# Order of matrix products and helper work in the expert part of an attention and expert kernel on one Trainium2 core

## The reference

```python
def _moe_ref(x, w_gate, w1, w2):            # x (2304, 512), 8 experts, F = 1024
    logits = x @ w_gate
    logits = logits - logits.max()
    P = np.exp(logits)
    for _ in range(8):
        P /= P.sum(1, keepdims=True) + 1e-09
        P /= P.sum(0, keepdims=True) + 1e-09
        P *= N / E
    for e in range(E):
        h = np.maximum(x @ w1[e], 0.0)
        ye = h @ w2[e]
        out += P[:, e:e + 1] * ye
```

## Time and profile before

| | us |
|---|---|
| median of 3 runs (lowest, highest) | 1875.57 (1874.74, 1875.81) |
| the profiled execution: its time | 1877.03 |
| the profiled execution: its span | 1874.8 |
| TensorE busy (share of the span) | 1854.2 (99%) |
| weight loads, beside the matmuls | 1601.0 (85%) |
| GpSimd busy | 1077.7 (57%) |
| VectorE busy | 978.2 (52%) |
| ScalarE busy | 760.3 (41%) |
| granted TensorE clock, mean share of full speed | 0.997 |

### The profile page before, as it was taken

How to read it: one execution, slowest core, us unless ns; L and a number is a source line. 1 busy time by engine, 2 the same in 40 slices (tenths; PEclk the granted TensorE clock), 3 DMA queues, 4 the chain that set the end, 5 groups by cost and what they waited for, 6 DMA issues and landing times.

```text
span 1874.8 us, 27897 instructions
## 1 busy us (share of the span) xinstructions
PE 1854.2 (99%) x10255; PEld 1601.0 (85%) x10255; DVE 978.2 (52%) x1846; ACT 760.3 (41%) x1314; POOL 1077.7 (57%) x720
## 2 busy tenths in 40 slices
PE   8999999899999999999999999999999999999999
PEld 4677777688999999998999999999989999999998
DVE  8877777757543444346434443444464434444443
ACT  8776777433333333334333333333333333333332
POOL 0223225456766666666676666666666666666662
PEclk9999999999999999999999999999999999999999
DMA  7753451111111111112111111111122111111110
GB/s 246 219 148 90 126 150 46 45 48 65 68 68 68 67 68 68 68 68 102 67 68 68 68 68 68 68 67 68 68 102 68 68 68 68 68 68 68 68 68 34
DMA packets 44160, 152.55 MB, mean 81 GB/s; under 512 B 9594, under 2 KB 18042, under 8 KB 29710
## 3 DMA queue, kind: packets, MB, share of 16 engines
q1 hardware_dynamic: 44046, 151.04, 24.9%
HBM read 135.69 MB, written 15.34 MB: 81 GB/s over the span
## 4 chain that ended last, share of the span: by engine, by line
PE 94%; DVE 2%; issue 0%; ACT 0%; DVEq 0%
PE banks L646 14%; PE banks L645 14%; PE banks L644 14%; PE banks L612 12%; PE banks L614 12%; PE banks L616 12%; PE banks L525 5%; PE banks L486 4%; PE banks L468 3%; PE banks L469 2%; PE banks L551 1%; PE banks L496 0%; DVE h_lo L1116 0%; DVE x_lo_first L1021 0%; PE banks L663 0%
## 5 line engine op out<-in xcount | busy, mean ns | idle before, releaser
L1224 POOL TENSOR_TENSOR w_lo<-stage,w_hi 128x1024 fp32r<-128x1024 f32 (+1 forms) x288 | 640.3, 2223 | 522.4 <-ACT w_hi L801 515.5
L646 PE MATMUL banks<-w_hi,h_lo 128*128 128x512 f32 x1152 | 455.1, 395 | 0.0
L612 PE MATMUL banks<-x_hi,w_hi 128*128 128x384 f32 x1344 | 452.3, 337 | 1.9 <-DVE u L1109 1.9
L645 PE MATMUL banks<-w_lo,h_hi 128*128 128x512 f32 x1152 | 453.8, 394 | 0.0
L616 PE MATMUL banks<-x_hi,w_lo 128*128 128x384 f32 x1344 | 451.5, 336 | 0.0
L644 PE MATMUL banks<-w_hi,h_hi 128*128 128x512 f32 x1152 | 448.0, 389 | 1.3 <-DVE h_lo L1116 1.3
L844 ACT ACTIVATE h_hi<-corner 128x384 fp32r<-128x384 f32 x288 | 150.0, 521 | 540.9 <-DVE corner L1109 540.9
L1109 DVE TENSOR_TENSOR corner<-u,banks 128x384 f32<-128x384 f32 x288 | 159.4, 553 | 386.6 <-PE banks L616 386.2
L801 ACT ACTIVATE w_hi<-stage 128x1024 fp32r<-128x1024 f32 (+1 forms) x288 | 282.3, 980 | 0.1
L612 PEld LDWEIGHTS banks<-x_hi,w_hi 128*128 128x128 f32 x1344 | 252.5, 188 | 18.4 <-DVE x_lo_rest L1021 2.2
L614 PE MATMUL banks<-x_lo_rest,w_hi 128*128 128x384 f32 x768 | 257.8, 336 | 0.0
(11 more groups left out here) (102 smaller groups left out, 2090.8 us busy)
## 6 DMA issues: line engine op xcount, KB each, us to landing
stage<-in_expert_w SPq DMA_DIRECT2D x96, 1024.0 KB, 4.7
raw<-in_qk SPq DMA_DIRECT2D x32, 576.0 KB, 7.2
bias_scratch<-bias_out SPq DMA_DIRECT2D x36, 288.0 KB, 2.7
bias<-bias_scratch SPq DMA_DIRECT2D x16, 288.0 KB, 2.7
v_main<-in_v SPq DMA_DIRECT2D x16, 256.0 KB, 2.6
bias<-bias_scratch SPq DMA_DIRECT2D x16, 256.0 KB, 3.6
out<-total SPq DMA_DIRECT2D x4, 768.0 KB, 4.1
out<-total SPq DMA_DIRECT2D x6, 256.0 KB, 2.0
```

The costliest lines, as they stand in the source:

```text
L612: pe.matmul(dst, hi[:, w, f], x_hi[:, k, c, :], start=fresh and c == 0, stop=False, skip_group_check=not fresh)
L645: pe.matmul(dst, h_hi[:, g % 2, f, tokens], lo[:, f], start=False, stop=False)
L646: mm = pe.matmul(dst, h_lo[:, g % 2, f, tokens], hi[:, f], start=False, stop=fp == FPAIRS - 1 and f == 1)
L1224: pool.tensor_tensor(lo, of, hi.bitcast(F32), ALU.subtract).then_inc(w_split, 1)
```

## The change

The second layer moves. In most periods the seven products stand in one run and the six tiles behind them (`TOGETHER`); periods 31, 32, 63, 64 and 95 keep the old places (`APART`). VectorE's list is rewritten for all periods: combinations first, then splits and additions. Product 2's bank is copied to a fourth block of `corner` by ScalarE, so product 4 waits for that copy alone, and hidden block 0 is rounded and split from the copy. ScalarE rounds the first weight piece after hidden block 0 and no longer ahead of it. Column totals and the two matmuls for the largest logit move behind tiles 0 and 3 of periods 1 to 6; they wait for the fourth combination of their period, and product 0 of the next period waits until VectorE has read them.

```diff
-TILES_AFTER = ((), (0, 1), (), (2, 3), (), (4,), (5,))
+APART = ((), (0, 1), (), (2, 3), (), (4,), (5,))
+TOGETHER = ((), (), (), (), (), (), tuple(range(TJ)))
...
-        TOTALS = [(3 + i // 2, 1 + 3 * (i % 2)) for i in range(ITERS)]
-        TOP_ROW = (1, 4)
-        TOP_ALL = (2, 1)
+        TOP_ROW = (1, 0)
+        TOP_ALL = (1, 3)
+        TOTALS = [(2 + (i + 1) // 2, 3 * ((i + 1) % 2)) for i in range(ITERS)]
...
+        def tiles_after(g, k):
+            changing = 0 < g < ALL and (g % PERIODS == PERIODS - 1 or g % PERIODS == 0)
+            return (APART if changing else TOGETHER)[k]
...
@@ product
+                    if g - 1 == TOP_ALL[0]:
+                        pe.wait_ge(top_neg, 1)
+                    if TOTALS[0][0] < g <= TOTALS[-1][0] + 1:
+                        pe.wait_ge(totals_kept, sum(t[0] < g for t in TOTALS))
...
                 elif k == 4:
-                    pe.wait_ge(h_split, 4 * g + 1)
+                    pe.wait_ge(corner_kept, g + 1)
...
+            def side_work(g, j):
+                if (g, j) not in [TOP_ROW, TOP_ALL] + TOTALS:
+                    return
+                pe.wait_ge(combined, 5 * g + 4)
...
@@ TensorE's loop
-                        for j in TILES_AFTER[k]:
+                        for j in tiles_after(g, k):
                             second_layer(g - 1, j)
+                            side_work(g, j)
...
+            def keep_corner(g):
+                act.wait_ge(product_done, NP * g + 3)
+                if g > 0:
+                    act.wait_ge(h_split, 4 * g - 3)
+                act.activation(corner[:, 0, :], product_bank(g, 0), ACT.Copy).then_inc(corner_kept, 1)
...
@@ ScalarE's loop
                 keep_first(g)
-                if more:
-                    round_weights(g + 1, 0)
-                if g == 1:
-                    place_logits()
                 if at == 0 and p > 0:
                     for k in range(4, NP):
                         round_factor(p, k)
+                keep_corner(g)
+                if g == 1:
+                    place_logits()
                 round_hidden(g, 0)
+                if more:
+                    round_weights(g + 1, 0)
...
@@ VectorE's loop, as it is now
                 combine(u2[:], product_bank(g, 1), p1_copy[:], ALU.add)
                 if at == 0 and p > 0:
                     for k in range(4, NP):
                         split_factor(p, k)
+                combine(u3[:], product_bank(g, 1), p1_copy[:], ALU.add)
+                combine(corner[:, 1, :], product_bank(g, 0), u3[:], ALU.add)
                 if g == 1:
                     largest_logit()
                 split_hidden(g, 0)
                 if after:
                     split_factor(p + 1, 0)
                     split_factor(p + 1, 1)
+                combine(corner[:, 2, :], product_bank(g, 1), u3[:], ALU.subtract)
+                combine(corner[:, 3, :], product_bank(g, 0), u2[:], ALU.add)
                 if after:
                     split_factor(p + 1, 2)
+                split_hidden(g, 1)
+                if g == 2:
+                    sinkhorn_rows(0)
+                read_side(g, 0)
+                add_tile(g - 1, 0)
                 split_hidden(g, 2)
                 if after:
                     split_factor(p + 1, 3)
+                add_tile(g - 1, 1)
                 split_hidden(g, 3)
+                add_tile(g - 1, 2)
+                read_side(g, 3)
+                for j in range(3, TJ):
+                    add_tile(g - 1, j)
```

More of the change, by code:

```diff
@@ L165, in bass_attention_moe @@
         h_hi = sb("h_hi", [P, 2, 2, 2 * T], F32R)
-        corner = sb("corner", [P, 3, T])
+        corner = sb("corner", [P, 4, T])
         h_lo = sb("h_lo", [P, 2, 2, 2 * T], F32R)
@@ L1074, in keep_totals @@
                 dve.wait_ge(col_all, k + 1)
-                link(dve.tensor_scalar(col_sum[:], banks[:, side(*TOTALS[k]), SIDE:SIDE + E], EPS, None, ALU.add))
+                dve.tensor_scalar(col_sum[:], side(TOTALS[k][0])[:, 0:E], EPS, None, ALU.add).then_inc(totals_kept, 1)
+                dve.wait_ge(totals_kept, k + 1)
             def sinkhorn_columns():
@@ L1114, in split_hidden @@
                 dve.wait_ge(h_rounded, 4 * g + i + 1)
-                source = product_bank(g, 0) if i == 0 else corner[:, i - 1, :]
-                dve.scalar_tensor_tensor(h_block(h_lo, g, f, part), source, 0.0, h_block(h_hi, g, f, part).bitcast(F32),
+                dve.scalar_tensor_tensor(h_block(h_lo, g, f, part), corner[:, i, :], 0.0, h_block(h_hi, g, f, part).bitcast(F32),
                                          ALU.max, ALU.subtract).then_inc(h_split, 1)
```

82 lines of the change are left out of this document (31 added, 51 removed).

## The result

| | before | changed kernel |
|---|---|---|
| median (lowest, highest), 4 executions each | 1875.69 (1874.74, 1876.62) | 1886.69 (1886.17, 1887.45) |
| ratio to before, 95% interval | | 1.0060 [1.0048, 1.0072] |
| profiled execution: time, span | 1877.03, 1874.8 | 1886.64, 1884.4 |

A forecast was written before the change was run, and what follows sets the result against it. TensorE's matmul spacings were taken as the bound. Terms -11.7 + 6.4 - 0.4 + 9.0 + 0.4 + 0.6 = +4.3, rounded to +4.4, on 1875.57 gave 1880.0 us; range 1870.5 to 1887.

The forecast's parts named there:

- What bounds the kernel: Expert part: TensorE, busy 99% of the span, hardly waits; the sum of its matmul spacings sets the end.
- Part 1: Plain periods: two runs instead of eight shorten 15.64 to 15.51 us without stalls; 90 periods, -11.7 us.
- Part 2: Helpers' work within a period: VectorE operations with SBUF operands end 0.03 to 0.41 us (768 columns: 0.81) after GpSimd's.
- Part 3: Routing, periods 2 to 6: blocked column steps stall TensorE, +6.4 us; period 0 gains 0.4.
- the old wait that went: Routing periods: the kernel before had a TensorE wait of about 0.6 us, forecast to go.
- Part 4: Periods 31/32 and 63/64: old TensorE order with VectorE's new list, (1.9 + 2.6) x 2 = +9.0 us.
- Part 5: Period 95: two splits instead of one needed before the last tiles start, +0.4 us.
- the 0.6 of restarts: Six new stops of TensorE, each costing some 0.1 us for restarting: +0.6 us.
- 1 (VectorE gets in ahead of GpSimd): Column step between tiles 0 and 3 takes its bare 2.4 us, no total waits: 1869.6 us; chance 0.18.
- 2: The run of seven products stalls, three combines each 0.05 us late in 90 periods: 1893.5 us; chance 0.08.
- 3: Regrouping saves nothing in plain periods, spacing depending on something else: 1891.7 us; chance 0.04.
- 4: The moved work doesn't move, VectorE's additions being overlapped differently than written: near 1875 us; chance 0.02.

The follow-up runs named there:

- experiment 8: Kernel before with 82 plain periods regrouped, but 63 of these have tiles in two groups of three, behind products 3 and 6; 1868.76 us, ratio 0.9965.
- run 173: Not a follow-up run: the words say that products 2 to 6 of the changed kernel take 173 ns a matmul.
- experiment 3: Changed kernel with GpSimd's weight sums of periods 1 to 8 and differences of periods 2 to 8 cut to 16 columns; 1877.07 us, ratio 1.0009.
- experiment 4: Changed kernel with sixteen unread 128-column matmuls filling TensorE's stop ahead of product 3 in periods 33 and 65; 1882.70 us, ratio 1.0038.
- experiment 7: Changed kernel with tiles of periods 9 to 94 outside the borders in two groups of three, behind products 3 and 6; 1926.4 us, ratio 1.0271.
- experiment 9: Changed kernel run again unchanged for a second trace; measured 1887.91 us.

## Why the prediction was right or wrong

**What bounds the kernel, and Part 1: right.** Gain by matmul spacings, 0.13 us a period and 15.51 for the new one; experiment 8 moves the number of groups alone and gets 15.57 for two. The prediction set against this a rule from the Trainium skill, page "TensorE: Matmul & The Clock Gate", section "Back-to-back issue gap": N/2.4 + 2.5 ns, with no term for what ran before. The section gives it for an isolated matmul. It doesn't hold for this stream, where the steady spacings are 173 and 227 ns and the first ones behind a change are longer. The hand-over margin of 0.12 us was enough everywhere: products 2 to 6 run 173 ns a matmul, as period 0 showed.

**Part 2: right in kind.** A split that reads `corner` is blocked by GpSimd: the mean rose from 823 to 1703 ns over all 384, and it is 0.55 where GpSimd is idle (experiment 3). Reading another source is only part of it. Split 0 went from 557 to 1614 ns, but the other three, which read `corner` before too, went from 912 to 1732, since they now stand beside GpSimd's differences. The Trainium skill says it, page "SBUF — State Buffer", section "Who interferes with whom": a VectorE operation with two SBUF inputs contends with a GpSimd operation that reads SBUF; one with a single SBUF input doesn't, unless it runs in a 2-port mode, which TENSOR_SCALAR can; and a reduction never does. The trace agrees on each: the split (two inputs) 1.83 and the scaling 2.07 in period 3, combinations, with one input in PSUM, 0.55, the TENSOR_SCALAR of `total` up to 2.62 instead of 0.47 in period 8, the reduction inside a sum 0.42.

**Part 3: right in mechanism, too small by 2.0 us.** Where it forecast stops they came, nearly of their size. In period 3 the step was done when forecast, at 14.42 for 14.4. That is partly luck: the forecast had three of its operations blocked, until 13.9. The trace has one, the column scaling, until 12.64, because GpSimd's differences ended at 12.47 and not at 11.9, and the step began 0.2 later; the rest ran nearly free beside the sums. And the price of passing on was left out: from the last partial total at 418.10 to tile 4 at 418.46, 0.36 us for the hand-over and two small matmuls. Product 0 of period 5 was 1.23 late (forecast 1.1), product 3 of period 5 1.19 (1.25). The same is missing in periods 2 and 4, 1.3 in all by the table. Missed: period 8, whose product 3 was 1.1 late for a forecast 0.1. The prediction gives no working for that 0.1; the six scalings of `total`, which read SBUF, wait there for GpSimd, and with GpSimd short the stop is gone (15.51, experiment 3). Periods 5 to 7, with the old wait that went, gave 0.4 back.

**Part 4: the step that failed in size.** Forecast 4.5 a border, measured 7.2 (with period 33 or 65 against 15.51):
- Period 31 to 32, product 0: 1.6 late, forecast 1.2. The second rest of an x factor ends 0.81 behind GpSimd's last difference, just as forecast, but that difference ends 15.8 us into the period and not 15.5 (`x_lo_first` in the waits).
- Tile 0 of 32: 0.75 on top, forecast 0.7.
- Product 3 of 33: the working had 7.1 us from product 6's end to the end of `u2`. Measured from 880.70 to 888.32 it was 7.6, so the stop was 3.16 and not 2.6. The three splits behind product 6 took 0.94, 1.05 and 0.46 to the next start where 0.47 each stood, so blocking by GpSimd is about 1.0 us of this stop; the rest is the six additions' place in the list. No run shortens GpSimd's work here.
- Behind it, 0.1 for restarting and 1.56 for the lower clock. The clock's term was missing: the prediction put the cost of a long stop at its length and 0.1. It is 3.1 of the 11.0 us, shown by experiment 4, which removes it and leaves the stop (-3.1 in the two periods, -4.0 in the medians).

**Part 5: right**, +0.47 for +0.4.

**The sum.** +4.4 became +11.0, 6.6 more: 3.1 from the clock, 2.2 from the borders' stops, 2.0 from the first eight periods and 0.1 from periods 0 and 95. Against that, the 0.6 of restarts is within the measured rows and comes off, and so does 0.3 of the plain periods, whose gain was 0.133 and not 0.13. The rest is rounding. The prediction's own terms add up to 4.3, so the 4.4 that it forecast with is 0.1 too high.

**The rivals.** 1 (VectorE gets in ahead of GpSimd) is dead: the column step of period 3 took 4.28 us (413.82 to 418.10) and not 2.4, and TensorE was 1.8 us late behind tile 3 in periods 3 and 4. 2 and 3 are dead by the 15.51. 4 also. The conditions for being wrong did not occur: the period is 15.51, and the new stops sum to some 22 us, within 8 to 25.

**The range** held the time by 0.3 us only, and that is luck as much as judgement. Its upper end came from independent errors of the terms, while three of them shared one cause (how long VectorE waits for GpSimd) and fell on the same side. And the 3.1 us of the clock, which it did not have, come or stay away from one execution to the next.

## What to carry to other kernels

A list of an engine and the order of the engine that it serves are one thing: change them together, place by place, and find the places where only one of them changed, for there the loss was (13.6 us here, against a gain of 10.7 in the 80 plain periods). When operations move from a free slot into one beside another busy engine, price each at "ends with the other's operation", sum these for the whole chain, and add the price of passing the result on (0.36 us here, two small matmuls included). A gain that holds in 80 like periods can be had alone: leave start, borders and end as they were.

## What the runs showed of the hardware

- **The clock falls at a stop of TensorE of about 3.3 us, but not each time.** With nothing in the stop it fell in 5 of 8 cases (2 of 2 in the changed kernel, 2 of 2 in its second trace, 1 of 2 in experiment 3, 0 of 2 in experiment 7), with filler matmuls in 0 of 2, and in none of the 19 stops of 2.0 us of experiment 7. It fell once behind a shorter one: product 3 of period 0 waits 1.56 or 1.94 us in all eleven traces, and only experiment 8 has a fall behind it. Each fall cost 1.4 to 1.6 us. Where it began varied too: 0.4 us ahead of the first matmul in period 33 of experiment 9, with the first matmul in the changed kernel's period 33, about 0.8 us later in its period 65, about 1.3 us later in experiment 3. What decides between falling and not in equal stops was not settled. The two windows of experiment 7 in period 33 show the same stop without a fall:

```profile
896.50:899.70 3.20, 0.24 (x2) 0.00 (x0) 3.18 (x6) 2.69 (x4) 1.67 (x2) 1.00 0.48 188
899.80:903.40 3.60, 3.60 (x17) 3.16 (x18) 0.56 (x1) 0.00 (x0) 3.09 (x2) 1.00 1.04 344
```

- **Blocking works in both directions.** GpSimd's three differences of period 3 took 7.20 us where the earlier trace rows sum to 1.85 + 2.41 + 2.41 = 6.67.
- **Changing from products (384 columns) to tiles (512) and back costs 0.067 us**, 26 ns on the first product and 29 and 12 on the first two tiles, without any wait in the trace; back from a single tile it costs less. Whether the column count does it or the other operands that change with it, no run separates.
